# Attention at the end of a unit: first scores per batch, value blocks split 5, 5, 5, 3, inverse sums earlier in DVE's program, operand splits one unit ahead

## What is computed

```python
def _attn_ref(q, k, v, w1, b1, w2):
    scores = scale * np.matmul(q, k.transpose(0, 1, 3, 2))     # 4 batches, 8 heads, 576 positions, 64 wide
    ...
    scores = scores + bias.transpose(2, 0, 1)[None, :, :, :]   # a bias for each head from relative positions
    scores = scores - np.max(scores, axis=-1, keepdims=True)
    attn = np.exp(scores)
    attn = attn / (np.sum(attn, axis=-1, keepdims=True) + 1e-09)
    return np.matmul(attn, v).astype(np.float32)
```

## Time and profile before

| | |
|---|---|
| median of three runs | 977.2 us (977.13 to 978.53) |
| the profiled execution | 981.7 us, span 979.9 us |
| attention, units 0 to 15 | first addition 56.8, last unit's first addition 297.6 us |
| busy over the span | PE 90%, DVE 56%, ACT 35%, POOL 34% |
| mean granted clock of TensorE | 0.955 |

### The profile page before, as it was taken

One profiled execution on the slowest core, in us unless ns is written; L12 is line 12 of the kernel. 1 busy time (PEld: TensorE's weight loads), 2 busy tenths in 40 slices (PEclk: granted clock), 3 DMA queues, 4 the chain that ended last, 5 costly groups with the idle time before them and its releaser, 6 DMA issues.

```text
span 979.9 us, 24926 instructions
## 1 busy us (share of the span) xinstructions
PE 882.6 (90%) x9749; PEld 761.0 (78%) x9749; DVE 544.2 (56%) x1004; ACT 340.4 (35%) x750; POOL 337.6 (34%) x346
## 2 busy tenths in 40 slices
PE   6867888888887359999999999999999999999998
PEld 3446677676776248888888888889999999999997
DVE  7986788888886665444444574446423333323331
ACT  7965576766765513321000241133211111111100
POOL 0617754423321178844000484487320202010100
PEclk9977899999999669999999999999999999999999
DMA  4779677677664686643000363454210202000001
GB/s 157 259 238 242 169 214 195 166 187 200 176 153 118 216 285 200 214 132 108 23 22 22 119 190 122 119 173 134 91 66 1 65 1 65 1 33 1 33 1 33
DMA packets 71472, 121.08 MB, mean 124 GB/s; under 512 B 26632, under 2 KB 30872, under 8 KB 69352
## 3 DMA queue, kind: packets, MB, share of 16 engines
q1 hardware_dynamic: 48360, 74.20, 26.3%
q10 hardware_dynamic: 17616, 30.27, 10.5%
q0 software_dynamic: 5424, 15.58, 5.0%
HBM read 93.12 MB, written 26.90 MB: 122 GB/s over the span
## 4 chain that ended last, share of the span: by engine, by line
PE 61%; POOL 2%; issue 1%; DVE 1%; DMA 0%; ACT 0%; ACTq 0%; POOLq 0%
PE moe_banks L1500 23%; PE moe_banks L1421 13%; PE moe_banks L1455 13%; PE moe_banks L1517 8%; PE moe_banks L1439 2%; POOL slots L1236 2%; PE moe_banks L1406 1%; PE moe_banks L1483 1%; DMA x_behind<-x_rows_by_tile,source 0%; POOL x_tok L1270 0%; DVE in_lane L1589 0%; ACT x_tok L1348 0%; PE moe_banks L1388 0%; POOL x_behind L1246 0%; ACT slots L1326 0%
## 5 line engine op out<-in xcount | busy, mean ns | idle before, releaser
L1236 POOL TENSOR_TENSOR slots<-x_tok,slots 128x512 fp32r<-128x512 f32 (+1 forms) x116 | 141.0, 1249 | 155.2 <-ACT slots L1326 155.0
L1500 PE MATMUL moe_banks<-yT,slots 128*128 128x384 f32 x1080 | 193.2, 334 | 0.0
L1500 PEld LDWEIGHTS moe_banks<-yT,slots 128*128 128x128 f32 x1080 | 187.9, 188 | 0.6
L1326 ACT CAST slots<-x_tok 128x512 fp32r<-128x512 f32 (+1 forms) x116 | 67.9, 602 | 254.7 <-PE moe_banks L1421 128.3
L1421 PE MATMUL moe_banks<-slots,xT 128*128 x600 | 147.5, 403 | 1.3 <-issue 1.3
L1455 PE MATMUL moe_banks<-slots,hT 128*128 x600 | 140.2, 389 | 0.6 <-POOL slots L1236 0.6
L784 ACT ACTIVATE probs<-probs,negmax 128x576 f32<-128x576 f32 x144 | 110.7, 770 | 78.3 <-DVE negmax L732 77.7
L1421 PEld LDWEIGHTS moe_banks<-slots,xT 128*128 128x128 f32 x600 | 113.9, 193 | 25.5 <-issue 1.9
L1455 PEld LDWEIGHTS moe_banks<-slots,hT 128*128 128x128 f32 x600 | 112.6, 188 | 24.2 <-issue 0.9
L732 DVE CUSTOM_DVE_ANT_0 probs<-s_ps,bias 128x576 f32<-128x576 f32 x144 | 103.3, 750 | 47.6 <-PE s_ps L634 44.7
L656 PE MATMUL o_ps<-pT,v_raw 32*64 32x160 f32 (+1 forms) x4608 | 110.1, 320 | 9.4 <-issue 7.5
(11 more groups left out here) (169 smaller groups left out, 990.5 us busy)
## 6 DMA issues: line engine op xcount, KB each, us to landing
x_tok<-in_moe_w ACTq DMA_DIRECT2D x96, 256.0 KB
v_raw<-in_v SPq DMA_DIRECT2D x64, 288.0 KB, 5.7
bias_table<-staged SPq DMA_DIRECT2D x36, 296.0 KB, 3.4
bias<-bias_table SPq DMA_DIRECT2D x32, 288.0 KB, 3.9
result_rows<-y SPq DMA_DIRECT2D x25, 256.0 KB, 2.1
q_raw<-in_q SPq DMA_DIRECT2D x16, 320.0 KB, 3.8
k_raw<-in_k SPq DMA_DIRECT2D x16, 288.0 KB, 3.2
x_rows_by_tile<-x_tok SPq DMA_DIRECT2D x16, 288.0 KB, 3.4
```

The costliest lines, as they stand in the source:

```text
L1236: nc.gpsimd.tensor_tensor(rest, raw(n, rows), near.bitcast(F32), ALU.subtract).then_inc(part_done(e, part)[0], 1)
L1326: nc.scalar.copy(near, raw(n, rows)).then_inc(near_done, 1)
L1500: last = nc.tensor.matmul(u_ps[m], final_weight(far, slots, m, d, a, f), yT[:, c, d, :], start=(d == 0 and k == 0), stop=(d == KD - 1 and ...
```

## The change

On PE the first scores of a unit are issued batch by batch (`first_scores`): batch 0 waits for the shared tile's addition alone, batch 1 for the copies of `x_ps` too. `VALUES` gives 5, 5 and 5 blocks to steps 0 to 2, none to step 3 and 3 to step 4, behind the next unit's first scores. On DVE `invert` stands behind the last turn of its own unit and ahead of the next addition. On ACT `store_output` stands between the exponentials of the two first tiles, and the near copies of the following unit are made in steps 0 and 1. On POOL the rests of the following unit stand ahead of `scale_outputs`, where before those of the unit two ahead stood behind it.

```diff
@@ -324,7 +324,7 @@
 
         STEPS = COMB + 1
 
-        VALUES = {0: range(0, 6), 1: range(6, 11), 2: range(11, 14), 3: range(14, KEY_BLOCKS)}
+        VALUES = {0: range(0, 5), 1: range(5, 10), 2: range(10, 15), 4: range(15, KEY_BLOCKS)}
 
         EPS = 1e-9
         INF = float(np.finfo(np.float32).max)
@@ -560,6 +560,11 @@
                 nc.gpsimd.tensor_tensor(rows, rows, inv[:, u, :].unsqueeze(2).broadcast_to([P, TILES, DH]),
                                         ALU.mult).then_inc(x_scaled, 1)
 
+            def rests_of_next(it, u):
+                following = (it, 1) if u == 0 else (it + 1, 0)
+                key_rests(*following)
+                query_rests(*following)
+
             def early_chunk(n):
                 _, near, rest = early_weights[n]
                 slot = n % SHORT_RING
@@ -581,9 +586,8 @@
             pool.wait_ge(gate_w_in, 16)
             nc.gpsimd.tensor_copy(turn_gate[:, :, 0:GATE], gate_w[:, :, 0:GATE])
             nc.gpsimd.tensor_copy(turn_gate[:, :, TURNED:], gate_w[:, :, GATE:]).then_inc(gate_placed, 1)
-            for u in range(2):
-                key_rests(1, u)
-                query_rests(1, u)
+            key_rests(1, 0)
+            query_rests(1, 0)
             token_bias(pool)
             pool.wait_ge(one_set, 1)
             for it in range(1, 3):
@@ -591,14 +595,13 @@
                     n = SHORT_RING * (it - 1) + 2 * u
                     early_chunk(n)
                     early_chunk(n + 1)
+                    rests_of_next(it, u)
                     scale_outputs(it - 1, u)
-                    key_rests(it + 1, u)
-                    query_rests(it + 1, u)
             with pool.Fori(3, HEADS - 1) as it:
                 for u in range(2):
+                    rests_of_next(it, u)
                     scale_outputs(it - 1, u)
-                    key_rests(it + 1, u)
-                    query_rests(it + 1, u)
+            rests_of_next(HEADS - 1, 0)
             for it in range(HEADS - 2, HEADS):
                 for u in range(2):
                     scale_outputs(it, u)
@@ -610,10 +613,8 @@
             def scores(it, u, s):
 
                 if s == 0:
-                    pe.wait_ge(k_rest, unit(it, u) + 1)
-                    pe.wait_ge(q_rest, unit(it, u) + 1)
-                    if not (isinstance(it, int) and unit(it, u) < 3):
-                        pe.wait_ge(x_copied, unit(it, u) - 2)
+                    first_scores(it, u)
+                    return
                 tiles = score_tiles(it, u, s)
                 for _, slot, count, _ in tiles:
                     pe.wait_ge(biased[slot], count)
@@ -636,6 +637,23 @@
                             if ends and half == 1:
                                 last.then_inc(scored[slot], 1)
 
+            def first_scores(it, u):
+
+                pe.wait_ge(k_rest, unit(it, u) + 1)
+                pe.wait_ge(q_rest, unit(it, u) + 1)
+                for b, slot, count, _ in score_tiles(it, u, 0):
+                    pe.wait_ge(biased[slot], count)
+                    if b == 1 and not (isinstance(it, int) and unit(it, u) < 3):
+                        pe.wait_ge(x_copied, unit(it, u) - 2)
+                    lanes = slice(b * DH, (b + 1) * DH)
+                    for n, (a, c) in enumerate(PASSES):
+                        ends = n == len(PASSES) - 1
+                        for half in range(2):
+                            keys = slice(half * HALF, (half + 1) * HALF)
+                            last = nc.tensor.matmul(s_ps[:, slot, half, 0:HALF], qT[u][a][lanes, 0:P], kT[u][c][lanes, keys],
+                                                    start=(n == 0), stop=ends)
+                    last.then_inc(scored[slot], 1)
+
             def values(it, u, blocks):
 
                 n = unit(it, u)
@@ -754,31 +772,29 @@
 
             def head(it, first, last):
                 for u in range(2):
-                    previous = (it, 0) if u else (it - 1, 1)
                     for s in range(STEPS):
                         if not (last and u == 1 and s == COMB):
                             add_bias(*after(it, u, s))
-                        if s == 0 and not (first and u == 0):
-                            invert(*previous)
                         turn(it, u, s)
+                    invert(it, u)
 
             bias_vector(dve)
             add_bias(0, 0, 0)
             heads_loop(dve, head)
-            invert(HEADS - 1, 1)
             for n, (_, near, rest) in enumerate(first_weights):
                 dve.wait_ge(near_done, HALF_LOADS + n + 1)
                 nc.vector.tensor_tensor(rest, stage[:, n % SHORT_RING, :], near.bitcast(F32), ALU.subtract).then_inc(w1_done, 1)
 
         @block.scalar
         def _(act):
-            def exponentials(it, u, s):
+            def exponentials(it, u, s, batches=(0, 1)):
                 step, _ = step_slot(it, u, s)
-                if s == 0 and not (isinstance(it, int) and it == 0 and u == 0):
+                if s == 0 and batches[0] == 0 and not (isinstance(it, int) and it == 0):
 
                     act.wait_ge(inv_done, unit(it, u) - 1)
                 for b, slot, count, tile in score_tiles(it, u, s):
-
+                    if b not in batches:
+                        continue
                     act.wait_ge(biased[slot], count + 1)
                     row = probs[:, step, b * SEQ:(b + 1) * SEQ]
                     nc.scalar.activation(row, row, ACT.Exp,
@@ -827,14 +843,17 @@
 
                         if s == COMB - 1 and not first:
                             copy_output(it - 1, u)
-                        if s == COMB and not (first and u == 0):
-                            store_output(*previous)
-                        if not (last and u == 1 and s == COMB):
+                        if s == COMB:
+                            if not (last and u == 1):
+                                exponentials(*after(it, u, s), (0,))
+                            if not (first and u == 0):
+                                store_output(*previous)
+                            if not (last and u == 1):
+                                exponentials(*after(it, u, s), (1,))
+                        else:
                             exponentials(*after(it, u, s))
-                        if first and u == 0 and s in (1, 2):
-                            (key_nears, query_nears)[s - 1](0, 1)
-                        if s >= COMB - 1 and not last:
-                            (key_nears, query_nears)[s - (COMB - 1)](it + 1, u)
+                        if s < 2 and not (last and u == 1):
+                            (key_nears, query_nears)[s](*(it, 1) if u == 0 else (it + 1, 0))
 
             def after_step(act, s):
                 if s in NEAR_AT:
```

## The result

| | before | changed |
|---|---|---|
| median of 4 runs each, us | 977.87 (977.13 to 983.16) | 1000.81 (999.16 to 1002.74) |
| ratio, with 95% interval | | 1.0228 (1.0206 to 1.0250) |
| profiled execution, us | 981.69 | 999.16 |
| its span, us | 979.9 | 997.4 |

The change makes the kernel 2.3% slower. The forecast was slower as well, but at 985.5 us, with a range up to 994: 1000.8 lies outside. The profiled execution of before was one of its longer ones and that of the changed kernel its shortest, so the spans differ by 17.5 us where the medians differ by 22.9.

The account below looks back on a forecast made before the run. No engine is full; DVE is nearest, so what makes it wait counts. Heads 2 to 6 +11.8, head 1 -0.6, head 7 -1.8, first two units -1.1 give +8.3 on the 977.2 us median: 985.5, range 974 to 994.

Parts of the forecast that it names:

- unit with values in time: Two batches of one head in the new order: 14.0 us, 0.8 less than now.
- A: Start of a unit's first addition on DVE, from which the forecast counts its times in us.
- values' first block begins: PE's first value block in a head's second unit: values land at A + 20.7, wanted at A + 17.3.
- clock, a head: Half clock on PE behind the wait for values, without cover: 1.7 us a head, bounds nothing and 3.3.
- the edits put at nothing: Counted at no cost: batch-by-batch scores (0.8 us a unit, covered by PE's idle time), POOL's new order, ACT's store between exponentials.
- 31.3 + 1.7: Length of each of heads 2 to 6: 31.3 us with late values plus 1.7 for the clock, +2.35 each.
- The lateness: Values late once a head behind splits and SP's queue: 3.3 us on a head of 28.0, making 31.3.
- Late values, half clock twice as long: Rival: PE's stretch after the wait too thin to raise the clock; +3.95 us a head, 993.5 us; chance 0.15.
- The likeliest case: Late values, then one fall of the clock: 985.5 us, own range 979 to 991, chance 0.55.
- The small terms: Everything outside heads 2 to 6: head 1 -0.6, head 7 -1.8, first two units -1.1; -3.5 us together.
- behind unit 14 (head 7's -1.8): Head 7 loads no keys, so its values are in time: first unit 15.8 to 14.0 us, -1.8.
- first two units: Start of the stage: one junction, and splits that stand two steps earlier; -1.1 us.

Follow-up runs that it names:

- e1: Changed kernel, but SP loads the values of each head's first unit before it waits for the second unit's splits: 972.97 us, 0.9899 of before.
- e4: Changed kernel with 24 unused matmuls on PE ahead of its wait for the values of a head's first unit: 999.27 us, 1.0139 of before.
- e5: Changed kernel with the splits where they were and first scores of both batches side by side again: 978.97 us, 0.9969 of before.
- e6: Changed kernel with the old splits and the inverse sums back between step 1's addition and step 0's turn: 986.47 us, 1.0047 of before.
- e9: Inverse sums back between addition and turn, on the changed kernel with values loaded ahead of SP's wait: 974.59 us, 0.9917 of before.
- e2: Kernel before with the moved splits alone, PE's and DVE's programs unchanged: 1006.14 us, 1.0218 of before.
- e10: Changed kernel with SP loading the first unit's values behind the splits' wait but ahead of the keys and queries: 985.11 us, 1.0044 of before.

## Why the forecast was wrong: point by point

The steps of the forecast, in head 4 (first addition at 197.67) and over heads 2 to 6:

| step | forecast | head 4 | heads 2 to 6 |
|---|---|---|---|
| unit with values in time | 14.0 | 14.08 | 14.05 to 14.09, 15.25 in head 2 |
| batch 1's first addition | A + 1.4 | A + 1.26 | |
| SP asks for keys | A + 11.2 | A + 11.35 | 11.3 to 11.4, 12.4 in head 2 |
| SP asks for values | A + 12.2 | A + 12.4 | 12.4, 13.2 in head 2 |
| values' first block begins | A + 20.7 | A + 20.98 | 20.9 to 22.3, mean 21.58 |
| PE's wait there | 3.4 | 3.75 | 3.7 to 5.1, mean 4.1 |
| head, values in time | 28.0 | | 27.84 (e1) |
| head, late values at full clock | 31.3 | | 32.05 (with e4) |
| clock, a head | 1.7 | | 2.3 |
| head | 33.0 | 33.71 | 34.39 |

The mechanism was foreseen: the chain of splits, SP's queue, landing and wait is there, and e1 shows that it is the cause, since with the values out of that queue the loss is gone. The array time of one batch after the other, 1.05 us a unit where 0.8 was taken, lay under PE's idle time, as forecast (e5), and the edits put at nothing cost nothing that shows in the units of 14.05 to 14.09 us. Two terms of the sum "31.3 + 1.7" were too small, and in the second the mechanism was off as well.

**The lateness: 3.3 forecast, 4.2 measured (32.05 - 27.84).** The forecast took 8.4 us, the longest landing in the earlier trace rows, from the first value load and put the landing at A + 20.7. In heads 4 and 5 that is nearly right; in head 6 it comes 0.7 us later and in heads 2 and 3 1.6 later. In head 2 the first unit takes 15.25 us and SP asks 0.8 us later for the values: DVE's inverse sums last 1.25 us there instead of 0.13, from 130.23 to 131.48, since POOL is splitting early expert weights (130.17 to 131.45), the hold that e6 and e9 show; where they take 0.13 us (e1) the unit takes 14.11. In head 3 SP asks in time, but the four loads have landed only 9.85 us behind the first request, in head 4 after 8.55; why was not tried. That 8.4 fits head 4 is luck in part: the load that comes last is the fourth, asked for 1.4 us behind the first, and it takes 7.2 us.

**The clock: 1.7 forecast, 2.3 measured.** "Today's fall costs 15.81 - 14.82 = 1.0 us with cover; without it I take 1.7" supposed one stretch of 3.4 us at half clock, as the earlier trace rows show it. There were two, one behind the other, in each of heads 2 to 6, and the first began while PE was still waiting:

| head | block begins | PE busy in the first slow stretch | from the block to the next head | of it the clock's (less 10.47) |
|---|---|---|---|---|
| 2 | A + 22.26 | 2.61 of 3.41 | 12.99 | 2.5 |
| 3 | A + 22.31 | 1.44 | 12.55 | 2.1 |
| 4 | A + 20.98 | 2.05 | 12.73 | 2.3 |
| 5 | A + 20.93 | 2.52 | 12.96 | 2.5 |
| 6 | A + 21.42 | 2.27 | 12.83 | 2.4 |

In the second stretch PE is busy all of the time in each. The less of the first is left when the values land, the cheaper it is. Head 1 of the same kernel is the case that the forecast had in mind: its wait is as long (4.13 us), but the clock falls at 114.89, 0.3 us behind the block's start, PE is busy all through that one stretch, and the clock is back behind it. e2 has two stretches in each of these heads too, the first with PE busy for 0.23 us at most, so that it slows next to no work.

The text named this as a rival, "Late values, half clock twice as long. PE's stretch after the wait could be too thin to raise it", at 993.5 and a chance of 0.15. That was the case that happened. Its head, 31.3 + 3.3 = 34.6, comes close to the 34.39 measured, but by luck: its price for the clock was 1.0 too high and its lateness 0.9 too low. The likeliest case had laid the wait from A + 17.3 to A + 20.7 and only then the half clock, and what a fall that begins inside the wait does was not worked out.

Heads 2 to 6 make 7.0 us of the miss. The small terms, forecast at -3.5 together and measured at -1.4, make 2.1:

| | forecast | profiles |
|---|---|---|
| heads 2 to 6 | +11.8 | +18.8 |
| head 1 | -0.6 | -1.1 |
| behind unit 14 (head 7's -1.8) | -1.8 | -0.3 |
| first two units | -1.1 | 0.0 |
| sum | +8.3 | +17.5 |

Head 7's first unit has its values in time, as forecast, but took 17.82 us, where 15.8 was to become 14.0:

```profile
299.52:317.34 17.82, 15.12 (x352) 12.66 (x352) 12.99 (x29) 10.67 (x30) 4.99 (x8) 0.90 0.43 101
```

It holds a stall of PE of 2.0 us that no other instruction ends ("issue" in the waits), and half clock behind it. The first two units hold another one, 4.14 us before 84.59, where before has 2.84. By profiles the change costs 17.5 us against 8.3 forecast; the medians say 22.9. The 5.4 us between lie in which executions were profiled, and no mechanism is behind them that a run shows: before's was 3.8 us above the median of its four runs beside it, the changed kernel's 1.7 below its own.

**Open.** Why PE stops for 2 to 4 us without a releaser in the first and last units of this stage, and why the parts outside heads 2 to 6 differ by up to 8 us between kernels that differ little there (67.8 to 75.0 us from unit 0 to unit 4, 697.9 to 705.7 behind unit 14; e4's filler is a part of its 75.0 and 702.6), was not tried. Nor is it known why the fall of the clock took one stretch in head 1 and two in heads 2 to 6, except by what PE did in the first: busy throughout in the one case, for 1.4 to 2.6 of 3.41 us in the other.

## What to carry to other kernels

Before moving work that a queue waits for, list what stands behind that wait in the queue: here four value loads stood behind a wait for splits that they had no need of, and another order of SP's requests turned 1.0228 into 0.9899. When a wait opens that starves TensorE, work out two prices, the wait at full clock and the slow stretch that begins inside it, and count the second from where it begins, not from where the wait ends; filling the wait (e4) shows the two apart. Where a head is paced by a chain that starts at its own first addition, work saved elsewhere in the head only lengthens the wait (e2).

## What was unforeseen in the hardware

- A VectorE instruction of 0.13 us (TENSOR_SCALAR on 128x9) lasts until GpSimd's running TENSOR_TENSOR ends: 1.50 us in e6, 0.62 in the earlier trace rows, 0.17 in e9 with GpSimd idle. In a profile it looks like busy time of DVE, not like a wait. VectorE's addition keeps its 0.75 us beside the same GpSimd instruction.
- Nearly the same wait of 1.6 to 1.8 us was followed by half clock in two heads of e10 and not in the other three, at 1.5 us a fall.
- In heads 2 to 6 of the changed kernel the clock stayed at half for a second stretch of 3.4 us; PE was busy 1.4 to 2.6 us in the first of the two and all through the second. In head 1, busy all through the first, it came back at once.
